# Attention by pairs of heads ahead of a two-layer feed-forward product: five steps for two heads, both tails in one block

## The reference

```python
scores = scale * np.matmul(q, k.transpose(0, 1, 3, 2))          # (4, 8, 576, 576), head_dim 64
bias = slopes[:, None, None] * (-np.abs(rel))[None, :, :]        # rel = pos[:, None] - pos[None, :]
mask = (rel >= 0) & (rel < 128)
scores = np.where(mask, scores + bias[None], -1000000000.0)
attn = np.exp(scores - np.max(scores, axis=-1, keepdims=True))
attn = attn / (np.sum(attn, axis=-1, keepdims=True) + 1e-09)
x = np.matmul(attn, v)                                           # then (2304, 512)
h = x @ moe_w_in;  g = h * (1.0 / (1.0 + np.exp(-1.702 * h)));   y = g @ moe_w_out
h = y @ moe2_w_in; g = piecewise(h);                             out = g @ moe2_w_out
```

## Time and profile before

| | |
|---|---|
| median of 3 runs | 887.19 us (886.96 to 887.35) |
| the profiled execution's own time | 886.86 us |
| its span, first to last instruction | 885.1 us |
| PE busy | 868.4 us (98%), 5804 matmul records |
| DVE, ACT, POOL busy | 708.1, 551.7, 116.5 us |
| granted TensorE clock | 1.000 |

### The profile page before, as it was taken

One profiled execution on the slowest core, in us unless ns is written; L12 is line 12 of the kernel. 1 busy time (PEld: TensorE's weight loads), 2 busy tenths in 40 slices (PEclk: granted clock), 3 DMA queues, 4 the chain that ended last, 5 costly groups with the idle time before them and its releaser, 6 DMA issues.

```text
span 885.1 us, 16377 instructions
## 1 busy us (share of the span) xinstructions
PE 868.4 (98%) x5804; PEld 849.4 (96%) x5804; DVE 708.1 (80%) x1052; ACT 551.7 (62%) x966; POOL 116.5 (13%) x85
## 2 busy tenths in 40 slices
PE   5999999999999999999999999999999999999998
PEld 4999888999999999999999999999999999999998
DVE  5777777567698886676997987988989779889794
ACT  4777887676775555667664547676556476765431
POOL 3667889400000000000000000000000000000000
PEclk9999999999999999999999999999999999999999
DMA  9987885177766643667867465388654653788822
GB/s 221 235 215 214 214 219 145 41 261 258 256 258 211 232 176 137 260 236 278 324 209 273 169 213 199 136 298 313 218 203 155 238 203 133 272 290 311 292 85 72
DMA packets 63654, 191.85 MB, mean 217 GB/s; under 512 B 7520, under 2 KB 14560, under 8 KB 59744
## 3 DMA queue, kind: packets, MB, share of 16 engines
q1 hardware_dynamic: 63584, 190.93, 64.7%
HBM read 118.55 MB, written 72.35 MB: 216 GB/s over the span
## 4 chain that ended last, share of the span: by engine, by line
PE 93%; POOL 3%; issue 1%; DVE 1%; DMA 1%; ACT 1%; SPq 0%; POOLq 0%; DVEq 0%; ACTq 0%
PE ps L964 78%; PE ps L925 6%; PE ps L889 4%; PE ps L906 3%; POOL qk_hi L777 1%; POOL k_lo L774 1%; PE ps L938 1%; DMA qk_raw<-qkT 1%; POOL w_first L801 0%; POOL arena L806 0%; DVE wst L1459 0%; PE ps L945 0%; POOL raw_first L829 0%; DVE w_first L1466 0%; DVE w_rest L1466 0%
## 5 line engine op out<-in xcount | busy, mean ns | idle before, releaser
L964 PE MATMUL ps<-arena,w_first 128*128 128x384 f32 x1764 | 331.8, 336 | 0.9 <-ACT ps L1198 0.8
L964 PEld LDWEIGHTS ps<-arena,w_first 128*128 128x128 f32 x1764 | 310.6, 188 | 2.4 <-issue 1.5
L964 PE MATMUL ps<-arena,w_rest 128*128 128x384 f32 x1260 | 240.8, 337 | 0.9 <-ACT ps L1198 0.8
L964 PEld LDWEIGHTS ps<-arena,w_rest 128*128 128x128 f32 x1260 | 220.1, 188 | 2.0 <-issue 1.7
L1518 DVE TENSOR_TENSOR arena<-raw_first,arena 128x768 fp32r<-128x768 f32 (+1 forms) x116 | 150.8, 1313 | 78.3 <-ACT arena L1168 78.2
L1168 ACT ACTIVATE arena<-raw_first 128x768 fp32r<-128x768 f32 (+1 forms) x120 | 131.9, 1117 | 46.4 <-DVE raw_first L1503 38.8
L964 PE MATMUL ps<-w_rest,arena 128*128 128x256 f32 x945 | 132.4, 281 | 0.0
L964 PEld LDWEIGHTS ps<-w_rest,arena 128*128 128x128 f32 x945 | 121.1, 189 | 0.1
L964 PE MATMUL ps<-w_first,arena 128*128 128x256 f32 x567 | 88.0, 282 | 0.0
L1118 ACT ACTIVATE probs<-probs,neg_max 128x256 f32<-128x256 f32 (+2 forms) x160 | 74.4, 468 | 16.1 <-DVE neg_max L1419 14.2
L1518 DVE TENSOR_TENSOR arena<-raw_rest,arena 128x1536 fp32r<-128x1536 f32 (+1 forms) x48 | 71.4, 1487 | 12.1 <-ACT arena L1168 12.0
(11 more groups left out here) (95 smaller groups left out, 955.8 us busy)
## 6 DMA issues: line engine op xcount, KB each, us to landing
gd<-g SPq DMA_DIRECT2D x24, 1536.0 KB, 6.1
raw_rest<-gd SPq DMA_DIRECT2D x32, 768.0 KB, 5.0
qk_raw<-qkT SPq DMA_DIRECT2D x64, 288.0 KB, 5.4
wst<-w_pairs SPq DMA_DIRECT2D x32, 512.0 KB, 6.0
raw_first<-gd SPq DMA_DIRECT2D x16, 768.0 KB, 6.3
yd<-ust SPq DMA_DIRECT2D x6, 1536.0 KB, 6.4
wd<-ust SPq DMA_DIRECT2D x4, 1536.0 KB, 8.5
raw_first<-yd SPq DMA_DIRECT2D x4, 1536.0 KB, 7.7
```

What stands on the lines that cost most here:

```text
L964: last = nc.tensor.matmul(to, stationary, moving, start=start and n == 0, stop=n == len(steps) - 1, skip_group_check=True)
```

## The change

The unit becomes a step with two blocks, and a pair of heads has five steps instead of ten units: the two tails, block 0 of both heads, blocks 1 and 2 of the first, block 3 of the first with block 1 of the second, blocks 2 and 3 of the second.

- **Scores** of both blocks of a step lie in one bank (there are three banks now), and one count of each semaphore stands for both.
- **Tails**: each tail's scores are computed with 128 queries, so that its 64 rows land in its own half of the partitions; the bias is two instructions of 64 rows, then there is one exponential, two transposes and two value matmuls of 128 columns for both. No matmul has 64 rows any more.
- **Output**: one reciprocal and two multiplications a pair (`write_pair`), and two copies of 64 rows for the tail.
- **Lags** in steps: transposes 2, values 4, writing 5, transposes of the pair 6, their copy 7, tail 8 and 9.
- **Casts**: DVE casts heads 2q+4 and 2q+5 in two steps in a row, behind the last step of pair q and the first of pair q+1. DVE takes the remainders of heads 0, 1, 13, 19, 25, 29 and 31.
- **Start**: the first 384 columns of head 0 are loaded and rounded ahead of the others; PE runs 22 matmuls on zeros first, as soon as `cleared` is there.
- **Handover**: the last pair is transposed within the first `duo`, and POOL's weight work starts at head 9.
- PE, DVE and ACT are written out without loops.

```diff
-ORDER = (0, 1, 4, 2, 3)
-SCORE_RING = 4
-PROB_RING = 8
+ITEMS = ((), ((0, 0), (1, 0)), ((0, 1), (0, 2)), ((0, 3), (1, 1)), ((1, 2), (1, 3)))
+FIRST_ORDER = (2, 3, 4, 0, 1)
+ORDER = [(q, d) for q in range(PAIR_COUNT) for d in (FIRST_ORDER if q == 0 else range(STEPS))]
+SCORE_RING = 3
+DVE_HEADS = (0, 1, 13, 19, 25, 29, 31)
+WARM_UP = 22
@@ sync
+        load_first_operands(True)
+        sp.dma_start(bias_sb[:, 0], bias_table[:, 0]).then_inc(bias_in[0], 16)
+        load_first_operands(False)
+        sp.dma_start(ident[:], identity).then_inc(ident_in, 16)
+        for h in range(1, HEADS):
+            load_operands(h)
+            sp.dma_start(bias_sb[:, h], bias_table[:, h]).then_inc(bias_in[h], 16)
+            load_values(h - 1)
...
@@ gpsimd
+        for head in range(2, 2 * PAIR_COUNT):
+            if head not in DVE_HEADS:
+                split_head(head)
+            if head in (9, 10, 11):
+                add_weights(0, head - 9)
+            if head in (13, 14, 15):
+                split_weights(0, head - 13)
+            if head in (16, 17, 18):
+                add_weights(1, head - 16)
+            if head in (20, 21, 22):
+                split_weights(1, head - 20)
+            if head in (23, 24, 25):
+                add_weights(2, head - 23)
+            if head == 26:
+                sum_s1()
...
@@ tensor: scores(m)
+            if (q, d) == (0, 2):
+                pe.wait_ge(first_split, 2)
+            elif q == 0:
+                for head in (0, 1):
+                    pe.wait_ge(qk_split[head], 2)
+            elif d == 0:
+                for head in (2 * q, 2 * q + 1):
+                    pe.wait_ge(qk_split[head % SPLIT_RING], 2 * (head // SPLIT_RING) + 2)
+            for i, (e, blk) in enumerate(ITEMS[d] or ((0, 4), (1, 4))):
+                query0 = blk * P if blk < 4 else 4 * P - e * TAIL
...
@@ tensor: duo, D == 0
+                product_5(u, up, c, k, D, 0)
+                transpose_pair(PAIR_COUNT - 1)
+                product_6(u, up, c, k, D, 0)
+                product_5(u, up, c, k, D, 1)
+                transpose_pair_tail(PAIR_COUNT - 1)
+                pe.wait_ge(pair_tail_copied, PAIR_COUNT)
+                mark_written(5)
+                mark_written(6)
+                product_6(u, up, c, k, D, 1)
@@ tensor: the order
+        warm_up()
+        pe.wait_ge(ident_in, 16)
+        for m in range(ALL_STEPS + VALUE_LAG):
+            if m < ALL_STEPS:
+                scores(m)
+            for gi, (_, last_step) in enumerate(GROUPS):
+                if last_step == m - VALUE_LAG:
+                    weigh_values(gi)
+            if 0 <= m - TRANSPOSE_LAG < ALL_STEPS:
+                transpose_probs(m - TRANSPOSE_LAG)
...
@@ vector: bias_scores(m)
+            if q < BATCH_PAIRS and d in (2, 3, 0):
+                for e in range(2):
+                    dve.wait_ge(bias_in[h + e], 16)
@@ vector: the order
+        round_first(True)
+        round_first(False)
+        for m in range(ALL_STEPS + COPY_TAIL_LAG):
+            if (q := pair_at(m, WRITE_LAG)) is not None:
+                write_pair(q)
+            if m < ALL_STEPS:
+                bias_scores(m)
+            if m in (0, 1, 2):
+                round_head(m + 1)
+            if (q := pair_at(m, 0)) is not None and q + 2 < PAIR_COUNT:
+                round_head(2 * q + 4)
+            if (q := pair_at(m, 1)) is not None and q + 2 < PAIR_COUNT:
+                round_head(2 * q + 5)
...
@@ scalar: the order
+            for gi, (_, last_step) in enumerate(GROUPS):
+                if last_step == m - TRANSPOSE_LAG:
+                    copy_transposed(gi)
+            if m < ALL_STEPS:
+                exponentials(m)
...
```

645 lines of the change are left out of this document (292 added, 353 removed).

## The result

The changed kernel takes **899.2 us** (median of four, 897.5 to 900.6), the kernel before 887.3: a ratio of 1.0133 (95%: 1.0111 to 1.0154). It is 12 us slower, where 876.5 us and a range of 866 to 885 were predicted. The profiled execution took 900.2 us, with a span of 898.4.

A forecast was written before the change was run, and what follows sets the result against it. PE's own pace was taken to bound the attention at first, POOL later. Terms 21.7 + 1.0 + 124.1 + 6.5 + 4.0 + 5.2 + 2.0 = 164.5 against 174.8 us, 10.3 sooner: 876.5 us, range 866 to 885.

The forecast's parts named there:

- Remainders on DVE: Five later heads' remainders on DVE make block 0's transposes late, 1.3 us each: 6.5 us (4.5 to 9).
- POOL: Weight instructions between two heads' remainders delay the next pair's scores behind heads 14, 16, 22, 26: 4 us (0 to 8).
- Rival C: In DVE's queue behind the first cast, DVE and POOL exclude each other all the time: 895 us, chance 0.07.
- Middle: Attention after pair 1's start: 1128 records at 0.110 us, 124.1 us if nothing waits; a pair takes 8.0 us.
- two heads take 5.8 us and fit: POOL's remainders of a pair's two heads, after a cast ending at 2.9 us, fit within 9.6 us.
- Start: Pair 1 starts at 21.7 us with some 40 records run instead of 65; 1 us added for slow records behind.
- Handover: From attention to first products: 5.2 us for products and marks as before, plus 2 us of new waits (0 to 4).
- A: In the attention nothing stands in PE's way and late steps are caught up: 865 us, chance 0.14.
- B: In the attention's pairs the DMAs set the pace: 884 us, chance 0.10.
- D: At the tails, the excess of 0.37 us stays despite the change: 888 us, no change, chance 0.07.

The follow-up runs named there:

- best order: Changed kernel with heads 13, 19, 25, 29, 31 on POOL, weight work reordered, earlier start, new writing, tails' copies on ScalarE, 30 more zeros: 874.4 us, ratio 0.9862.
- order_only: Changed kernel with only heads 13, 19, 25, 29, 31 moved to POOL, and weight instructions, ScalarE's roundings and DVE's first sums reordered: 880.6 us, ratio 0.9921.
- best_dve: The best order with remainders of heads 13, 19, 25, 29 and 31 back on DVE: 897.0 us, ratio 1.0123.
- dve01: Changed kernel with DVE taking remainders of heads 0 and 1 only, all other heads on POOL: 902.8 us, ratio 1.0170.
- pool_order: Changed kernel with POOL's weight instructions only behind odd heads, up to three in a pair with a head on DVE: 905.1 us, ratio 1.0194.
- both: Changed kernel with POOL's weight instructions cut to 8 columns and all heads from 2 on split by POOL: 901.4 us, ratio 1.0154.
- best_late: The best order with the changed kernel's start (first bias waits for both tables, head 3 on POOL, no further zeros): 878.0 us, ratio 0.9903.
- fill_waits: Changed kernel with 96 transposes of the identity filling eight of PE's waits in the middle: 897.9 us, ratio 1.0124.
- best_spare: The best order with DVE also filling two spare buffers behind the casts of heads 13, 19, 25, 29 and 31: 878.4 us, ratio 0.9892.
- light_pool: Changed kernel with POOL's weight instructions on 8 columns only, two fillings of their buffers ahead: 898.9 us, ratio 1.0126.

## Why the prediction was wrong

The mechanism of the gain was right: fewer records, PE at one every 0.11 us. The best order reaches at 163.2 us the point that was predicted for 164.5. What was wrong is the terms that pay for it. Two of them failed by about as much, the one that turned the gain into a loss first.

**"Remainders on DVE", 6.5 us (4.5 to 9), and "POOL", 4 us (0 to 8)**: this is the step that failed. The five heads and the order around them are worth 18.6 us (order_only; 21.0 between the two profiled spans), against 10.5 for both terms; the heads alone, put back into the best order, cost 22.6. Without them the kernel is faster, if less than forecast. I let DVE's lateness work against block 0's transposes, with 1.1 us to spare, and took 1.3 us a head. The order on DVE shows what stands behind the remainders as well: the pair's copy, and PE's tail transpose waits for it with all else behind. I also gave the waits of both remainders 0.9 us a head (1.8 less 0.9) at most, where they lost 1.6 on average (15.6 us against 7.6), and 2.0 at head 19 in best_dve. The measured price is 4.1 to 4.5 us a head in the best order (20.4 in span, 22.6 by the medians, over five). In PE's waits of the changed kernel it does not show so plainly: 6.6 us ahead of L932 and 8.0 at pair starts. It shows in the pairs, 10.4 to 12.2 us with such a head against the 9 to 10 that were forecast. Rival C named the exclusion, with 1.5 us for a DVE head and three waits of up to 1.4: 5.7 us. Its mechanism and its 895 us were near to what happened; 0.07 was far too little for it.

**The two terms are not a sum.** Taking heads off DVE alone gained nothing (dve01, 3.6 us slower, with overlapping intervals), moving POOL's weights alone made it 5.9 slower (pool_order), and order_only, which does both, is 18.6 faster. I costed each with the other engine standing still. pool_order shows the point by itself: POOL's waits went and DVE's grew. dve01 shows it less cleanly, since its late waits come from ScalarE's first operands; order_only also moves ScalarE's roundings, DVE's first sums and the third weight, and has another table than pool_order. How much is the meeting of both engines and how much these other moves is not shown.

**Middle, "a pair is 73 x 0.110 = 8.0 us"**: the count was right, the pace too good. In the cleanest pairs it is 8.53 us; over the pairs of order_only it is 8.67, so 0.64 x 15 = 9.6 us more than 73 x 0.110 = 8.03. That is as large an error as the one above (18.6 less 10.5 is 8.1, in span 10.5). The step that failed here is "two heads take 5.8 us and fit". In the run both, from the start of a pair's last step (103.40) the first cast ended after 3.1 us (2.9 forecast), and POOL's two heads ended 6.8 us behind it (5.8 forecast), since one of its remainders of 64 rows takes 1.81 us beside the second cast. So the scores came 9.9 us from there and not 9.6. In order_only ten of thirteen pairs start 0.1 us behind POOL as well. DVE's share of a pair (7.5 us measured, 7.6 to 8.0 predicted) was right; it sets when POOL gets its cast. With 0.45 us of tails' copies off DVE, plain pairs take 8.1 to 8.3. No run shortens POOL's remainders alone, so this part is read from the traces and not tested.

**Start**: 23.3 us against 21.7. The wait of the first bias for head 1's table was in the forecast (9.8 us, measured 10.3). What was not is that POOL began head 2 at 16.5 us instead of 15.4 and took 3.3 us a head instead of 2.8, since its remainders of 64 rows needed 1.80 us each beside DVE's casts. Behind it 32 records from 23.28 to 29.96 us took 6.68 at a granted clock of 0.51; at 0.110 they take 3.5, so 3.2 us where 1.0 was given. The old start as a whole costs 3.6 us against the new one (best_late).

**Clock**: for the middle I gave nothing. It fell in five stretches, which cost 1.3 to 2.7 us (fill_waits); they are part of the 21.

**Handover and the part behind**: near enough. The waits at the first products were 2.3 us in all, where 2.0 was given, 1.5 of them behind the last marks; that is most of what the part behind is longer.

So the 23.6 us are about 10.5 for heads and POOL's order (21.0 in span against 10.5), 9.6 for the pace of pairs, 1.6 for pair 1's start and 2.2 for the records at half clock behind it: 23.9. It is an account and no proof: the 21.0 are two single executions, and the medians give 18.6. Without the two terms the forecast is 154.0 us and order_only's trace has 167.1, 13.1 more, where 9.6 + 1.6 + 2.2 is 13.4; but the 9.6 comes from that same trace. Rivals A, B and D did not happen. DMA's share in the middle was 0.66, and the cleanest pairs ran at 1.05 without a cast waiting. No record with 64 rows was left, and none of its excess.

What stays open: how much of a head's 4 us on DVE is exclusion and how much load. best_spare puts the load at 4.0 to 5.6 us of 20 to 22, but with fillings, and with POOL doing the remainders too; it is no bound.

## What to carry to other kernels

When work moves between two engines that hold each other up, cost them as one queue: list what stands behind the moved instruction on its engine, take each of the instructions at its length beside the other engine, and follow the last one to the engine that waits. Test moves of such work together as well as alone, since here neither half by itself was a gain and the whole, with the roundings moved to match, was one of 19 us. And a new order has waits of its own (data that has not landed, a load queued behind another's wait) that hide what it brings until they are found in the trace.

## What the runs showed of the hardware

- DVE's remainder (two SBUF inputs, 0.76 us free) took 1.66 us on average and up to 1.85 beside POOL's. The Trainium skill (SBUF — State Buffer, Who interferes with whom) says that such an instruction and a GpSimd one that reads SBUF exclude each other, and that the one that comes second waits for the whole of the other. The prediction had no row for two inputs; these rows agree. With a wait at the cast and at both remainders, as rival C had it, the term would have been above its upper end.
- DVE's cast, with one SBUF input, waits as well (1.49 and 1.85 us for 0.76), and not only for a POOL instruction that reads: in the runs light_pool and both a smaller cast took 6.0 and 6.1 us for 0.56 and ended 0.4 us behind a filling on POOL. A filling on DVE keeps its 0.54 us beside POOL.
- POOL pays too: its remainder of 64 rows took 1.81 us where DVE's cast ran ahead of it, and 1.41 alone.
- Of two waits of PE that are equally long, one is followed by half clock (97.60, 1.77 us), the other is not (90.11, 1.74 us, granted clock 1.00 from 90.1 to 94.0). And behind the wait that ended at 92.08 (best_dve) the records are slow at once, while behind the one at 97.60 the next three scores still ran at full pace.
